# Scores of each head over its own 64 rows, means of the first pair computed first, and an unused product in 25 tiles

## The reference

```
# attention: a window of 16 positions to each side, and 24 block summaries
k_sum = k.reshape(B, H, 24, 32, D).max(axis=3)
v_sum = v.reshape(B, H, 24, 32, D).mean(axis=3)
scores_l = where(|i - j| < 16, scale * q @ k.T, -1e9)
scores_s = scale * q @ k_sum.T + log(32)
a = softmax(concat([scores_l, scores_s]))       # denominator + 1e-9
x = a @ concat([v, v_sum])                      # then (B, 768, 512)
# mixing over positions, then over channels
u = x + (relu(x.T @ w_tok1) @ w_tok2).T
y = u + relu(u @ w_ch1) @ w_ch2
# normalised MLP
out = y + relu(layernorm(y) * g @ w2_ch1) @ w2_ch2
```

## Time and profile before

| | us |
| --- | --- |
| median of 3 runs | 611.28 |
| lowest, highest | 610.35, 612.75 |
| the profiled execution, its own time | 612.84 |
| span of its trace | 611.1 |
| TensorE busy | 594.0 (97%) |
| VectorE, ScalarE, GpSimd busy | 219.8, 159.4, 49.6 |

### The profile page before, as it was taken

The page is one execution under the profiler, slowest core; times in us unless marked ns, Lnnn a source line. Parts: engine busy times, 40 slices in busy tenths (PEclk is TensorE's granted clock), DMA queues, the critical chain, the costliest instruction groups (busy, mean ns, idle before and its releaser), DMA issues.

```text
span 611.1 us, 7428 instructions
## 1 busy us (share of the span) xinstructions
PE 594.0 (97%) x2808; PEld 484.1 (79%) x2808; DVE 219.8 (36%) x537; ACT 159.4 (26%) x331; POOL 49.6 (8%) x91
## 2 busy tenths in 40 slices
PE   6899999999999999999999999999999999999997
PEld 2677888878888788878888788888788888788886
DVE  5387666466334311134533632112521113211112
ACT  3376664334323101113332310112111102101110
POOL 5356541000000000000000000000000000000000
PEclk9799999999999999999999999999999999999999
DMA  8877532014333000000223100000100000100001
GB/s 231 226 210 225 168 106 96 17 35 137 104 104 104 1 0 1 0 1 8 96 103 104 34 2 2 0 1 0 70 0 1 0 1 0 70 1 0 1 0 69
DMA packets 21305, 35.58 MB, mean 58 GB/s; under 512 B 7596, under 2 KB 7832, under 8 KB 21272
## 3 DMA queue, kind: packets, MB, share of 16 engines
q1 hardware_dynamic: 20720, 34.69, 18.5%
q10 hardware_dynamic: 552, 0.44, 0.3%
HBM read 31.39 MB, written 3.15 MB: 57 GB/s over the span
## 4 chain that ended last, share of the span: by engine, by line
PE 92%; DVE 3%; issue 2%; DMA 2%; ACT 1%; POOL 0%; SPq 0%; DVEq 0%; ACTq 0%; POOLq 0%
PE bank L367 88%; PE bank L516 1%; DMA k_sb<-k_w 1%; DVE neg_scores L725 1%; DMA v_far<-v_mean 1%; PE bank L400 1%; PE bank L402 1%; PE bank L401 1%; DVE k_sb L713 1%; ACT probs L594 0%; DVE natural L844 0%; POOL v_tree L328 0%; ACT tok_w L610 0%; DVE x_split L707 0%; DVE natural L738 0%
## 5 line engine op out<-in xcount | busy, mean ns | idle before, releaser
L820 DVE SCALAR_TENSOR_TENSOR hidden<-bank,hidden 128x512 fp32r<-128x512 f32 x84 | 58.1, 691 | 309.3 <-ACT hidden L644 309.3
L367 PE MATMUL bank<-slots_late,hidden 128*128 128x512 f32 x648 | 156.4, 391 | 0.0
L644 ACT ACTIVATE hidden<-bank 128x512 fp32r<-128x512 f32 x84 | 50.2, 598 | 353.7 <-PE bank L367 353.7
L367 PEld LDWEIGHTS bank<-slots_late,hidden 128*128 128x128 f32 x648 | 120.9, 188 | 24.7
L367 PE MATMUL bank<-in_t,slots_late 128*128 128x512 f32 x576 | 137.7, 389 | 1.1 <-issue 1.1
L367 PEld LDWEIGHTS bank<-in_t,slots_late 128*128 128x128 f32 x576 | 107.9, 188 | 24.5 <-issue 2.3
L367 PE MATMUL bank<-in_t,slots_early 128*128 128x512 f32 x288 | 69.5, 390 | 0.0
L367 PEld LDWEIGHTS bank<-in_t,slots_early 128*128 128x128 f32 x288 | 54.1, 188 | 11.7
L367 PE MATMUL bank<-slots_early,hidden 128*128 128x512 f32 x216 | 51.9, 389 | 0.0
L367 PEld LDWEIGHTS bank<-slots_early,hidden 128*128 128x128 f32 x216 | 40.5, 188 | 8.4
L367 PE MATMUL bank<-k_sb,q_sb 128*128 128x364 f32 x96 | 39.7, 499 | 4.2 <-DVE neg_max L725 2.5
(11 more groups left out here) (72 smaller groups left out, 430.0 us busy)
## 6 DMA issues: line engine op xcount, KB each, us to landing
stage<-w_ch SPq DMA_DIRECT2D x56, 256.0 KB, 2.7
k_sb<-k_w SPq DMA_DIRECT2D x16, 273.0 KB, 4.2
v_own<-v_w SPq DMA_DIRECT2D x8, 390.0 KB, 3.1
q_sb<-q_t SPq DMA_DIRECT2D x8, 384.0 KB, 4.9
v_turned<-v_t SPq DMA_DIRECT2D x8, 384.0 KB, 3.7
out<-natural SPq DMA_DIRECT2D x12, 256.0 KB, 2.1
tok_stage<-w_tok SPq DMA_DIRECT2D x4, 384.0 KB, 4.0
v_far<-v_edge SPq DMA_DIRECT2D x16, 45.0 KB, 2.9
```

The costliest lines, as they stand in the source:

```text
L367: return nc.tensor.matmul(dst, lhs, rhs, start=start, stop=stop, skip_group_check=True)
L644: nc.scalar.activation(hidden[:, f % HID_RING, 0, :], ch1_bank[f % 2][:, 0:GN], ACT.Relu).then_inc(hid_high, 1)
L820: nc.vector.scalar_tensor_tensor(out=hidden[:, f % HID_RING, 1, :], in0=ch1_bank[f % 2][:, 0:GN], scalar=0.0, in1=hidden[:, f % HID_RING, ...
```

## The change

The scores of a tile are made head by head, each in a product of 182 columns whose operands lie in 64 partitions: 0 to 63 for head 0, 64 to 127 for head 1. The zeros and their clearing go. `k_sb` has 206 columns a tile (24, window of 158, 24), loaded by one DMA for both heads. The three score banks hold one head each, so head h of tile n takes bank (2n + h) % 3 and waits for the mask three heads back. The key maxima of both heads come from one reduction over 128 partitions in the first round of a pair, into a tile of their own, and GpSimd copies them to all 6 tiles, twice 64 partitions.

For pair 0 VectorE sums the values by one reduction, TensorE transposes them after 13 of now 19 unused products, and ScalarE's queue sends the means before its first exponentials. The value tile v_turned of pair 0 is the first load of ScalarE's queue. The ones in `v_far` come by DMA, those at the window's edges with the edges themselves. In each round of n below 25 one unused product of 512 columns in bfloat16 stands between turning and weighing.

```diff
-SUM_AT = (WIN, 0)
-WIN_AT = (0, NSUM)
+SUM_AT = (NK, 0)
+KEYS_AT = (NSUM, 0)
-WARM = 16
+WARM = (13, 6)
...
-            k_sb = sb(a, "k_sb", [P, KB, 2, NT, NK])
+            k_sb = sb(a, "k_sb", [P, KB, NT, KW])
+            k_max = sb(a, "k_max", [P, 2, NSUM])
...
+        def send_means(queue, r):
+            i = r % 2
+            queue.wait_ge(mean_copied, r + 1)
+            if r >= 2:
+                queue.wait_ge(pv_done, NT * (r - 1))
+            else:
+                queue.wait_ge(ld_ones, 32)
...
             load_k(0)
             load_q(0)
-            load_turned(0)
             load_v(0)
             load_turned(1)
             load_k(1)
             load_q(1)
-            send_means(0)
             load_v(1)
...
-                    at = SUM_AT[h]
-                    ks = k_sb[64 * h:64 * h + 64, i, h]
-                    pool.wait_ge(kmax_done, 2 * r + h + 1)
-                    pool.sem_inc(pool_passed)
-                    nc.gpsimd.tensor_copy(ks[:, 1:NT, at:at + NSUM],
-                                          ks[:, 0:1, at:at + NSUM].broadcast_to([64, NT - 1, NSUM])
-                                          ).then_inc(k_ready, 1)
+                    half, at = slice(64 * h, 64 * h + 64), SUM_AT[h]
+                    pool.wait_ge(kmax_done, r + 1)
+                    nc.gpsimd.tensor_copy(k_sb[half, i, :, at:at + NSUM],
+                                          k_max[half, r % 2, :].rearrange("p (t n) -> p t n", t=1)
+                                          .broadcast_to([64, NT, NSUM])).then_inc(k_ready, 1)
...
-                if n >= 3:
-                    pe.wait_ge(scored, 2 * (n - 3) + 2)
-                mm(score_bank[n % 3][:, 0:2 * NK].rearrange("p (h k) -> p h k", h=2), q_sb[:, i, t * P:(t + 1) * P],
-                   k_sb[:, i, :, t, :], True, True).then_inc(qk_done, 1)
+                for h in range(2):
+                    if 2 * n + h >= 3:
+                        pe.wait_ge(scored, 2 * n + h - 2)
+                    half = slice(64 * h, 64 * h + 64)
+                    mm(score_bank[(2 * n + h) % 3][:, 0:NK], q_sb[half, i, t * P:(t + 1) * P],
+                       k_sb[half, i, t, KEYS_AT[h]:KEYS_AT[h] + NK], True, True).then_inc(qk_done, 1)
...
-            for _ in range(WARM):
+            for _ in range(WARM[0]):
                 mm(mix_bank[:], warm[:, 0:P], warm[:], True, True)
-            pe.wait_ge(k_clear, CLEARS)
+            pe.wait_ge(ld_ident, 16)
+            pe.wait_ge(init_done, 3)
+            turn_sums(0, mix_bank[:, mean_at])
+            pe.wait_ge(mean_copied, 1)
+            for _ in range(WARM[1]):
+                mm(mix_bank[:], warm[:, 0:P], warm[:], True, True)
...
                 if n + 1 < NTILE:
                     turn(n + 1)
+                if n < MIX0:
+                    mm(mix_bank[:], warm[:, 0:P], warm[:], True, True)
                 weigh(n)
...
-            act.dma_start(v_init[:], value_init).then_inc(ld_init, 16)
+            act.dma_start(v_turned[:, 0, :], v_t[0, 0]).then_inc(ld_vt[0], 16)
+            act.dma_start(ident[:], identity).then_inc(ld_ident, 16)
             act.dma_start(mask_sb[:], mask).then_inc(ld_mask, 16)
-            act.dma_start(ident[:], identity).then_inc(ld_ident, 16)
+            for i in range(2):
+                act.dma_start(v_far[TAIL:TAIL + 2 * NSUM, i], value_ones).then_inc(ld_ones, 16)
             act.dma_start(gain_sb[:], gain).then_inc(ld_gain, 16)
+            copy_means(0, mix_bank[0:NSUM, mean_at])
+            send_means(act, 0)
             exps(0)
             exps(1)
-            copy_means(0, mix_bank[0:NSUM, mean_at])
...
+            dve.wait_ge(ld_vt[0], 16)
+            dve.wait_ge(init_done, 1)
+            nc.vector.tensor_reduce(v_sum[:, 0, 0:NSUM], v_turned[:, 0, :].rearrange("p (n s) -> p n s", s=BLOCK),
+                                    AX_X, ALU.add).then_inc(vsum_done, 1)
+            key_maxima(0)
...
-                if t in (0, 1) and r + 1 < NPAIR:
-                    key_maxima(r + 1, t)
+                if t == 0 and r + 1 < NPAIR:
+                    key_maxima(r + 1)
```

102 lines of the change are left out of this document (37 added, 65 removed).

## The result

The changed kernel is slower than the one before. Four runs of it took 620.23, 655.49, 619.93 and 638.42 us, four of the kernel before on the same chip 610.35 to 614.38. The median of all four is 629.33. The forecast was 604.7.

The account below looks back on a forecast made before the run. TensorE's own work was taken as the bound from 24 us on, after a hole at the start. Terms -6.2, +1.0 and -1.4 sum to -6.6: profiled 612.84 becomes 606.2, median 604.7; range 600 to 621.

Parts of the forecast that it names:

- from tile 3 to tile 24: Weighing of tile 3 to that of tile 24: 38.3 us after against 37.33 before, +1.0.
- The start: Up to the weighing of tile 3: early means bring it to 19.7 us from 25.94, -6.2; tile 0 weighed at 14.0.
- The fourth rival: At the start: early means fail, the hole moves to pair 1's keys or the ones; 611, chance 0.12.
- The scores over 64 rows: Scores of each tile as four quarters of 182 columns, half the possible overlap taken: 0.07 us off a tile.
- Rivals 1 and 3: Full overlap of heads' scores: -0.15 a tile, 602, chance 0.14; a stop at each row change: +0.32, 620, chance 0.18.
- my low bound: Scores of a tile: two middle quarters run side by side, three quarters in a row, 0.46 us.
- my high bound: Scores of a tile: TensorE stops at both row changes, 0.32 us added to 0.61, giving 0.93.
- The unused product: Between turning and weighing in the first 25 tiles: nothing hides it, 0.21 us each, 5.3 in all.
- The token cast: Second head's scores wait for a late mask after a token cast: 0.25 us in each of four pairs, +1.0.
- The pair-start stall of 0.93: Wait before scores at pair starts: earlier key maxima make this stall of 0.93 us go.
- After tile 24: The 20 sets of scores behind tile 24: 20 x -0.07, -1.4 us.
- second rival: Clock falls within the first 25 tiles, 1.7 us more a tile; eight such tiles give +7, 618.5; chance 0.18.

Follow-up runs that it names:

- Experiment 4: The change with the start of before (16 unused products, GpSimd value sums, means by SP's queue), gain ahead of the mask, ones still by DMA: 615.41 us, ratio 1.0082.
- experiment 3: The kernel before with only the unused product of 512 columns added in each of the first 25 tiles: 612.58 us, ratio 1.0006.
- experiment 11: The kernel before with its scores as two products of 182 columns over all 128 rows instead of one of 364: 611.74 us, ratio 1.0006.
- Experiment 7: The kernel before with early means of pair 0 (VectorE sums, SP's queue, gain ahead of the mask), 128-row scores, no unused product in tiles: 609.9 us, ratio 0.9968.
- experiment 9: The kernel before with early means, both key maxima in a pair's first tile, token weights' low part a tile later: 608.56 us, ratio 0.9946.
- 13: As experiment 9, with the means of pair 1 issued ahead of the keys of pair 2: 612.16 us, ratio 1.0006.
- 17: As experiment 9, with the first two casts of token weights three and one tiles later: 610.82 us, ratio 0.9953.
- experiment 8: As Experiment 4, with both heads' scores from partitions 0 to 63 (head 1's output is another): 681.39 us, ratio 1.105.
- experiment 15: As 13, with the unused product in each of the first 25 tiles: 615.36 us, ratio 1.0071.
- 12: As experiment 6, token weights' low part a tile later: seven runs at 608.23 to 610.49 us (ratio 0.9962), six at 643.16 to 643.87.
- 10: As 5, with the low part of the token weights one tile later on VectorE: 615.22 us, ratio 1.0046.
- experiment 1: The change without its unused product in the first 25 tiles (the 19 at the start stay): 645.78 us, ratio 1.056.
- 2: The change with the gain's load moved ahead of the mask in ScalarE's queue: 651.95 us.
- 14: The change with ones by VectorE, pair 1's values ahead of pair 0's, means of pairs 0 and 1 by SP's queue ahead of the next keys: 652.96 us.
- 16: As 14, without the unused product in the tiles: 642.39 us, ratio 1.0505.
- 18: The change with transfers ordered by need, 17 first unused products, later token casts: five runs 613.13 to 616.4 us (ratio 1.0051), three 655.5 to 655.8.
- 5: The change with ones by a VectorE copy, gain early, means of pair 0 by SP's queue ahead of pair 1's keys: 614.61 us, ratio 1.0054.
- experiment 6: As 5, without the unused product in the first 25 tiles: 612.61 us, ratio 1.0.

## Why the prediction was wrong

The forecast's sum for the profiled execution was 606.2, and it took 620.2. The 14 us split by the landmarks into 8.9 at the start, 2.8 from tile 3 to tile 24, and 2.3 behind it.

**The start (forecast -6.2, measured +2.7) is the step that failed.** It said that the ones land at "about 9 us", that the means go out then and arrive after 5.1 us, as before, and that the first masks come 1.2 us after the scores; it had no term for the gain. The ones took 8.5 us from an issue at 2.17 and after, the gain 9.6 from its issue at 3.61, and from the issue of the means at 11.77 to the weighing that needs them were 9.3. I had taken the ones' landing from their queue's bytes at half the rate, and a transit time from a moment at which the queues were emptier: the DMA moved 335 to 361 GB/s from 6 to 18 us, against 308 and 205 before. Moving the sending of the means to ScalarE's queue, and the ones to a DMA, took away both waits at which SP's queue had stood, and its loads for pairs 1 and 2 went out ahead of the means. Experiment 4 has only the wait for the means back, with the same ones by DMA: there the means need 3.9 us, and tile 3 comes 5.0 us earlier. It moved the gain and the value sums as well, so how much of the 5.0 is that wait alone isn't shown. The sentence "I am wrong altogether if weighing 0 still stands behind 17 us" applied: 21.08. The fourth rival had the right mechanism (the hole moves to the ones) but no term for a longer one.

A second thing was uncertain in that step: its base was one trace. The kernels of experiments 3 and 11 have the start of before, and their traces weigh tile 3 at 24.22 (with the product) and 22.09 (without), not 25.94. At tile 24 experiment 11 is only 1.2 us ahead of the trace of before (62.07 against 63.27). So the 25.94 is not the same in every execution, and an earlier tile 3 gave little at tile 24 even in the old order.

Experiment 7 shows what early means give on 128-row scores: -0.3%; with two moves of VectorE's work beside them, experiment 9 has -0.5%. Their gain shrinks on the way, because tile 6 then comes before its own transfers do: in the traces of experiments 9, 13 and 17 a late transfer stops TensorE there for 3.6 to 5.7 us, whichever is put first.

**The scores over 64 rows (forecast -0.07 a tile, measured 0).** Rivals 1 and 3 were both true, and cancel. The overlap is 0.30, not the 0.15 of my low bound, which had let only the middle two of four quarters run side by side: all of the upper head's run beside all of the lower head's (experiment 8). Against it stand 0.10 ahead of the first quarter, 0.05 behind the first transpose, and 0.15 between the scores and that transpose (0.51 - 0.30 - 0.06, where before 0.67 - 0.61 = 0.06): 0.30 for two changes of rows, near the 0.32 of my high bound. The split rests on the overlap at full clock, which is halved from the lower one; that gain and cost cancel is measured. At the lower clock they don't: 0.91 us from the first score to the next transpose against 1.31 over 128 rows. Experiment 11 shows that it isn't the shorter instructions. The Trainium skill, TensorEngine Tiling (Array Packing), Key Properties, says that a change of the tiling mode drains TensorE; these runs agree, with an estimate of 0.15 us for each change from the 0.30 above. The same skill, TensorE: Matmul & The Clock Gate, "Part 3: Packing small matmuls", lets tiles in different row groups run at the same time; this too agrees, with the 0.60 of experiment 8. I had set two right rules against each other as alternatives, when they add.

**The unused product (forecast 0.21 a tile, 5.3 in all).** The 0.21 was right in the plain tiles of the change and of experiment 3. The total depended on what else waited: under 1 us on the kernel before (experiment 3, 612.58 against 611.84), 3.2 in experiment 15, 5.6 between experiments 12 and 10. In the change itself, whose pair-start stalls are gone, it came through whole: 21 x 1.82 + 3 x 0.11 + 4 x 0.64 = 41.1, and measured were 41.12.

**The token cast (forecast 0.25 in each of four pairs, measured 0.64).** Place and mechanism were right, the term was mis-sized by 1.6 us in all. I had moved the chain up by 0.3 to 0.4, and it moved by 0.10: the mask behind the low part starts 33.27 - 29.39 = 3.88 us after the scores of tile 7, before 41.57 - 37.59 = 3.98 after those of tile 13. And I had the second head due 0.3 after the first, but it runs beside it and is due with it: at 2 x 1.82 = 3.64, where it comes at 33.67 - 29.39 = 4.28. With 1.3 for the plain tile's 0.06 this makes the 2.8 of tiles 3 to 24. The pair-start stall of 0.93 did go.

**After tile 24 (forecast -1.4, measured +1.0 at tile 47 and +0.9 at the end):** a tile with mixing takes 75.85 - 73.49 = 2.36 us against 69.28 - 66.97 = 2.31, not 0.07 less but 0.05 more, over 23 tiles.

**The clock (second rival, 0.18).** It names what happened in two of four runs of the change, and in a way I hadn't thought of: I let it cost 1.7 us in each of four to eight tiles, and in the six profiled runs of such kernels that show it (1, 2, 12, 14, 16 and 18) it stays until the mixing has begun, between 91 and 111 us. In the traces of the change and of experiments 4 and 10 it comes back earlier, at 19 to 25 us. The argument against it ("the clock held 1.00 through waits of 1 us") was read on 128-row scores. Over all kernels with 64-row scores on rows of their own and the unused product, 14 of 42 runs have a mean clock below 0.96; without the product 17 of 27. Four pairs of kernels differ by the product alone: with and without it 2 and 4 of 4 (the change and 1), 0 and 1 of 4 (5 and 6), 1 of 8 and 6 of 13 (10 and 12), 4 of 4 and 6 of 6 (14 and 16). That points to a help, in part of the runs, and is no proof. Over all with 128-row scores, holes of 4 to 6 us included, none of 58, nor one of more than 90 runs of the kernel before. Experiment 8 differs from 4 only in the rows of the second head's scores and has four of four low, where 4 has one of ten. 16 against 13, and 31 of 69 runs against none of 58, tie it to the 64-row kernels; experiment 11 shows that two products in place of one are not enough for it. Why the chip grants it so, and whether such a stream would lose the clock with no hole before it, stays open.

## What to carry to other kernels

Before moving a step forward, list the transfers that it waits for, with the landing times of the trace, and count what the move lets into the queues ahead of them; here a 2 KB load behind 1.05 MB of its own queue landed 9.6 us after its issue. A wait that is taken away, or moved to another queue, also took care of order. And two rules about one instruction, a gain by overlap and a cost by a change of mode, are to be added before they are weighed against each other.

## What the runs showed of the hardware

A kernel whose scores are 64-row products can keep TensorE busy 70.00 of 70 us and stay at the lower clock (experiment 1), where the same work over 128 rows was back at the upper one by 34 us, after a hole of 4 to 6 us (experiments 9 and 13). At full clock the gain of two heads side by side and the cost of a change between 128 and 64 rows and back cancel (a plain tile of 1.61 us in either form, experiment 6), each about 0.30 us by the estimate above. Two fp32 products on separate halves of the rows ran side by side: 0.91 us against 1.51 at the lower clock (experiment 8).
